# Attention and two MLP layers on one core: another order of reads, loads and first products, and the second product six tiles behind

## The chip, the cores and the metric

The kernel runs on one core of a Trainium2 chip. The metric is the device time of one execution in microseconds: 915.09 before the change, the median of three runs (912.17 to 916.41).

## The reference

Three parts, one after the other. Attention with 2 batches, 8 heads, 768 positions and head size 64:

```python
scores = scale * np.matmul(q, k.transpose(0, 1, 3, 2))
is_global = pos[None, :] < int(n_global)                  # 8
is_local = (rel >= 0) & (rel < int(n_local))              # 96
dist = np.where(is_global & ~is_local, float(n_local), np.abs(rel))
scores = np.where(is_global | is_local, scores - slopes * dist, -1e9)
a = softmax(scores)                                       # over the keys
x = (a @ v), heads side by side                           # 1536 x 512
```

Then an MLP, `h = x @ w_in` (512 to 2048), `g = h * tanh(softplus(h))`, `x2 = g @ w_out`. Then four experts, each `relu(x2 @ w1[e]) @ w2[e]` (512 to 1024 to 512), weighted by normalized `domain_probs` and added.

## The kernel before

**Precision.** The large products are made of fp16 halves: a matrix is scaled by a power of two and split into a high and a low fp16 part, and a product is three matmuls (high x high, high x low, low x high). The scale needs a bound of the largest absolute value, so v, w_in and w_out are each read once for it before they are split.

**Attention.** There are 8 pairs of heads, 12 units in each (6 query tiles of 128 rows, 2 heads). A unit's keys are only the band: the tile before, its own and 32 global columns, 288 columns from the third query tile on, 128 and 256 in the first two. For a unit TensorE makes scores (L540, for two units at a time, three units ahead of use), VectorE adds the distance table and finds the row's extreme (`biased`, L1074, two units ahead), ScalarE takes the exponential (`expo`, L824, two ahead), TensorE transposes (`turn`, L566), ScalarE copies out a high half (L858), VectorE makes the low half (L1184), and TensorE multiplies with the values (`pv`, L585, two units behind). VectorE's `output` divides by the row sums in three small steps per half pair. `fill` (L497) transposes q and k of the next pair, ScalarE copies them out. Every engine's order is written out by hand in `pair`; engines meet at semaphores alone.

Beside this, at steps counted as `at` = 12 x pair + unit: VectorE reads |v| of one pair per unit of pair 0 (`value_step`, L1155). ScalarE reads |w_in| in eight pieces of 1024 columns at steps 21 to 28 and |w_out| at 33 to 40 (`weights_sum`, L841), as a sum of absolute values, which bounds the maximum. GpSimd then splits both matrices (`split_all`, from L745). x of the first 512 tokens is transposed during pairs 4 to 7 (`turn_x`, L505; ScalarE L893 and VectorE L1169 make the halves).

**Head.** SyncE loads the bounds, q and k of pair 0, v of pair 0, q and k of pair 1, then the other v. VectorE writes the identity, tests the bounds, and builds the distance table of 672 columns in eight steps (`distances` and two more, L1040 to L1052). The scores wait for all four copies of q and k of pair 0.

**First MLP.** 1536 tokens in 3 groups of 512, 16 tiles of 128 hidden columns: 48 steps T. In step T TensorE makes the first product of tile T (12 matmuls, `first_product`, L635) into one of four PSUM banks and, LAG = 4 tiles behind, the second product of tile T - 4 (12 matmuls, L658) into the other four. Between them stands the activation: ScalarE's exponential of T (L939), VectorE L1297, L1299, L1303, ScalarE's logarithm and exponential of T - 1 (L953, L955), VectorE L1315, L1317 for T - 1, GpSimd's product (L790), ScalarE's high half and VectorE's low half (L947, L1309) of T - 2. The hidden halves live in a ring of 8 tiles. The groups 1 and 2 of x are transposed in steps 0 and 2, before the first second product, through the banks that the second products use. When a group is done, ScalarE copies x2 out of PSUM (`take_x2`, L911); TensorE's next group waits for it. In ScalarE's order this copy stands at the start of step T = LAG + 16 x group:

```python
for T in range(STEPS + LAG):
    taken = x2_due(T, 0)
    if taken and taken[1] == 0:
        take_x2(taken[0])
```

After step 47 the loop's first products are those of expert 0.

Of the kernel before, what the change touches and what calls it, by code (L numbers as in the profile page):

```python
# [13 lines left out]
P = 128  # L14
# [22 lines left out]
def program(nc, q, k, v, n_global, n_local, w_in, w_out, probs, w1, w2, out):  # L37
# [35 lines left out]
    with ExitStack() as ctx:  # L73
# [103 lines left out]
        dist_b, key_b, loc_b = (scratch(BAND_COLS) for _ in range(3))  # L177
# [5 lines left out]
        rel_b, glo_b = dist_b, tmp[:, 3 * BAND_COLS:4 * BAND_COLS]  # L183
# [56 lines left out]
        w_piece = sem("w_piece")  # L240
# [53 lines left out]
        LAG = 4  # L294


        TURN_AT = {0: 1, 2: 2}
# [21 lines left out]

        W_LOAD_AT = UNITS + 6  # L320
# [16 lines left out]
        FILL = [(j, t) for j in range(2) for t in (range(HEAD), range(HEAD, QT))]  # L337
# [38 lines left out]
        def run_attention(eng, first, pair, rest):  # L376
# [18 lines left out]
            with eng.If(banded == 1):  # L395
                run(True)
                rest()
            with eng.Else():
                run(False)
                rest()  # L400
# [79 lines left out]
        def _(pe):  # L480
            def fill(i, slot, k, banded):
# [14 lines left out]
                for n, t in enumerate(tiles):  # L496
                    last = pe.transpose(psum(k if m_0 else 3, P, n * P), nat[slot][j][:, t * P:(t + 1) * P], ident[:])  # L497
# [10 lines left out]
            def score_parts(i, slot, u, banded):  # L508
# [3 lines left out]
                if u == 0:  # L512

                    pe.wait_ge(tr_out, FILLS * (2 * i + slot + 1))
# [73 lines left out]

            def pair(i, slot, banded):
                for u in range(UNITS):  # L590
# [34 lines left out]
            def rest():  # L625

                pe.wait_ge(o_ready, 2 * PAIRS + 2)

                def split_product(dst, lhs, rhs, chunks, fresh=None):

                    for c in range(chunks):
                        if fresh is not None:
                            fresh(c)
                        for n, (a, b) in enumerate(((0, 0), (0, 1), (1, 0))):
                            last = pe.matmul(dst, lhs(c, a), rhs(c, b), start=(c == 0 and n == 0),  # L635
                                             stop=(c == chunks - 1 and n == 2))
                    return last

                def first_product(T):

                    g, f = divmod(T, FT)
                    if T >= 4:
                        pe.wait_ge(b_ready, T - 3)
                    split_product(psum(T % 4), lambda c, s: w_in_s[:, s, c, f * P:(f + 1) * P],
                                  lambda c, s: xs(g, c, s), DC).then_inc(h_psum, 1)
# [51 lines left out]
                pe.wait_ge(x_ready, DC)  # L697
                pe.wait_ge(w_split, 1)
                for T in range(STEPS + LAG):
                    if T < STEPS:  # L700
# [3 lines left out]
                    if T in TURN_AT:  # L704
                        pe.wait_ge(x_ready, DC * TURN_AT[T])
# [13 lines left out]
            pe.wait_ge(ident_ready, 1)  # L719
            for k in range(FILLS):  # L720
# [85 lines left out]
        def _(act):  # L806
# [27 lines left out]
            def weights_sum(n, c):  # L834
# [6 lines left out]
                act.activation(scaled[:], src[:, c * PIECE:(c + 1) * PIECE], ACT.Abs,  # L841
                               accum_out=wpieces[:, c:c + 1]).then_inc(w_piece, 1)
# [7 lines left out]
            def pair(i, slot, banded):  # L850
                for u in range(UNITS):
# [28 lines left out]
                if not banded and not after(i, slot):  # L880
# [3 lines left out]
                    for c in range(PIECES):  # L884
# [11 lines left out]
            def rest():  # L896
# [79 lines left out]
            for k in range(FILLS):  # L976
                copy_out(0, 0, k, k)
# [4 lines left out]
        def _(dve):  # L982
# [23 lines left out]

            dve.wait_ge(bounds_in, 32)
# [15 lines left out]
            def weights_part(n, c):  # L1023

                if c in (0, PIECES // 2):
# [394 lines left out]
```

## Time and profile before

| | us |
|---|---|
| median of three runs | 915.09 |
| the profiled execution, time | 915.88 |
| its span, first to last instruction | 913.8 |
| TensorE busy in it | 873.1 |
| VectorE busy | 506.8 |
| ScalarE busy | 315.7 |
| GpSimd busy | 266.0 |

PE is TensorE's matmuls, PEld its weight loads, DVE VectorE, ACT ScalarE, POOL GpSimd, SP SyncE. A line number is that of the code above. Busy time is the time in which an engine works on an instruction; where an engine idles the trace tells how long and which instruction ended it. The attention takes the first 154 us, the first MLP to 423 us, the experts the rest.

### The profile page before, as it was taken

The page shows a single profiled execution, that of the slowest core. Times are in us where ns is not written, and L with a number is a line of the kernel's source. Part 1 is how long each engine was busy: PE and PEld are TensorE (multiplying, and loading weights), DVE is VectorE, ACT ScalarE, POOL GpSimd, SP SyncE. Part 2 cuts the span into 40 slices and gives each one's busy share as a digit, 9 for nine tenths or more (in the row PEclk, how much of TensorE's full clock was granted, in tenths as well). Part 3 has the DMA queues.
Part 4 walks back from the last instruction along what each step waited for, and adds up shares of the span by engine and source line. Part 5 has one row for each costly group of instructions (what it writes and reads, how often), then busy time and mean ns, then how long its engine had stood idle before and what let it go on. Part 6 is the DMA issues. An engine that isn't in the chain of part 4 may idle for free.

```text
span 913.8 us, 12568 instructions
## 1 busy us (share of the span) xinstructions
PE 873.1 (96%) x4884; PEld 441.3 (48%) x4884; DVE 506.8 (55%) x1016; ACT 315.7 (35%) x591; POOL 266.0 (29%) x218
## 2 busy tenths in 40 slices
PE   3878998999999999999999999999999999999998
PEld 3766786444444444444444444444444444444443
DVE  7855876999999999996642225322134322212121
ACT  3699885545454555454030111101020101101020
POOL 1266994122222232320009500059000193000000
PEclk8798999999999999999999999999999999999999
DMA  9762340000000000202000400000400000000001
GB/s 220 242 220 55 82 156 1 1 1 1 0 1 10 1 0 1 78 18 93 4 6 0 151 34 0 7 1 2 182 1 0 6 0 0 1 24 23 34 12 49
DMA packets 52005, 39.20 MB, mean 43 GB/s; under 512 B 40816, under 2 KB 41712, under 8 KB 51440
## 3 DMA queue, kind: packets, MB, share of 16 engines
q1 hardware_dynamic: 49888, 34.31, 12.5%
q10 hardware_dynamic: 2064, 4.19, 1.3%
q8 instruction: 31, 0.51, 0.3%
q14 instruction: 22, 0.18, 0.1%
HBM read 35.35 MB, written 3.15 MB: 42 GB/s over the span
## 4 chain that ended last, share of the span: by engine, by line
PE 69%; DVE 21%; ACT 7%; issue 2%; DMA 0%; POOL 0%; DVEq 0%; SPq 0%; ACTq 0%
PE bank L635 58%; PE bank L658 5%; DVE tmp L1299 4%; DVE tmp L1317 3%; PE bank L540 2%; DVE xT L1315 2%; DVE tmp L1297 2%; PE bank L566 2%; DVE tmp L1303 2%; ACT scaled L841 2%; PE bank L585 1%; DVE hid L1309 1%; ACT tmp L824 1%; ACT tmp L858 1%; ACT tmp L953 1%
## 5 line engine op out<-in xcount | busy, mean ns | idle before, releaser
L927 ACT ACTIVATE hid<-bank 128x512 f16<-128x512 f32 x96 | 57.3, 596 | 410.6 <-PE bank L635 410.6
L635 PE MATMUL bank<-xT,wA 128*128 128x512 f16 (+1 forms) x864 | 196.2, 381 | 1.1 <-DVE acc L1114 1.1
L1290 DVE SCALAR_TENSOR_TENSOR hid<-bank,hid 128x512 f16<-128x512 f32 x96 | 66.4, 692 | 172.3 <-ACT hid L927 172.3
L658 PE MATMUL bank<-hid,wB 128*128 128x512 f16 x576 | 132.2, 379 | 4.4 <-ACT acc L911 2.6
L635 PEld LDWEIGHTS bank<-xT,wA 128*128 128x128 f16 x864 | 84.8, 98 | 103.7 <-issue 2.2
L790 POOL TENSOR_TENSOR tmp<-tmp 128x512 f32<-128x512 f32 x48 | 70.1, 1460 | 198.2 <-DVE tmp L1317 198.2
L635 PE MATMUL bank<-wA,hid 128*128 128x512 f16 x576 | 125.3, 379 | 0.0
L635 PE MATMUL bank<-xT,wB 128*128 x576 | 125.3, 379 | 0.0
L635 PE MATMUL bank<-wB,hid 128*128 128x512 f16 x576 | 125.3, 379 | 0.0
L745 POOL TENSOR_SCALAR stage<-stage,sc 128x1024 f32<-128x1024 f32 x32 | 35.9, 1120 | 252.8 <-DVEq L1283 240.8
L1366 DVE SCALAR_TENSOR_TENSOR acc<-bank,pg,acc 128x512 f32<-128x512 f32 x36 | 27.0, 751 | 131.7 <-PE bank L635 131.7
L658 PEld LDWEIGHTS bank<-hid,wB 128*128 128x128 f16 x576 | 56.1, 98 | 73.0 <-DVE hid L1309 3.6
L635 PEld LDWEIGHTS bank<-wA,hid 128*128 128x128 f16 x576 | 56.4, 98 | 67.9
L635 PEld LDWEIGHTS bank<-xT,wB 128*128 128x128 f16 x576 | 56.4, 98 | 68.0
L635 PEld LDWEIGHTS bank<-wB,hid 128*128 128x128 f16 x576 | 56.4, 98 | 68.0
L947 ACT ACTIVATE hid<-tmp 128x512 f16<-128x512 f32 x48 | 30.2, 630 | 107.8 <-POOL tmp L790 106.0
L1184 DVE SCALAR_TENSOR_TENSOR tmp<-bank,tmp 128x384 f16<-128x384 f32 (+2 forms) x96 | 47.0, 490 | 30.5 <-ACT tmp L858 29.4
L635 PE MATMUL bank<-xT,hid 128*128 (+1 forms) x288 | 63.3, 379 | 0.0
L824 ACT ACTIVATE tmp<-tmp 128x288 f32<-128x288 f32 (+2 forms) x96 | 48.7, 507 | 20.3 <-DVE tmp L1074 18.8
L566 PE MATMUL bank<-ident,tmp 128*128 128x128 f32 x240 | 47.4, 299 | 6.0 <-DVE tmp L1184 3.3
L1299 DVE SCALAR_TENSOR_TENSOR tmp<-tmp 128x512 f32<-128x512 f32 x48 | 48.4, 1007 | 1.6
L540 PE MATMUL bank<-hid 64*128 64x256 f32 (+2 forms) x320 | 39.7, 360 | 9.1 <-DVE tmp L1074 8.2
(110 smaller groups left out, 930.6 us busy)
## 6 DMA issues: line engine op xcount, KB each, us to landing
stage<-in_moe_w SPq DMA_DIRECT2D x8, 2048.0 KB, 9.1
stage<-in_moe_w_in SPq DMA_DIRECT2D x1, 4096.0 KB, 14.2
wB<-in_moe_w_out ACTq DMA_DIRECT2D x1, 4096.0 KB, 15.9
hid<-in_q SPq DMA_DIRECT2D x16, 192.0 KB, 3.2
hid<-in_k SPq DMA_DIRECT2D x16, 192.0 KB, 3.4
xT<-in_v SPq DMA_DIRECT2D x8, 384.0 KB, 5.1
out_y<-acc SPq DMA_DIRECT2D x12, 256.0 KB, 2.0
rows<-max SPq DMA_DIRECT2D x4, 128.0 KB, 4.2
```

What stands on the lines that cost most here:

```text
L540: last = pe.matmul(*parts[a][n], start=True, stop=True)
L566: last = pe.transpose(dst[:, b * P:(b + 1) * P], src[:, b * P:(b + 1) * P], ident[:])
L635: last = pe.matmul(dst, lhs(c, a), rhs(c, b), start=(c == 0 and n == 0), stop=(c == chunks - 1 and n == 2))
L658: last = pe.matmul(psum(4 + d), w_out_s[:, a, f // 2, f % 2, d * P:(d + 1) * P], hv[:, T % RING, b, :], start=(f == 0 and n == 0), stop=(f ...
L745: pool.tensor_scalar(tmp, src, scale, 1.0, ALU.mult, ALU.mult).then_inc(w_part, 1)
L790: pool.tensor_tensor(g_t[T % 4], g_t[T % 4], r_t[T % 2], ALU.mult).then_inc(g_ready, 1)
L824: act.activation(t, t, ACT.Exp, bias=nmax[:, u:u + 1], scale=-1.0).then_inc(p_ready, 1)
L927: act.activation(hv[:, f, 0, :], psum(f % 4), ACT.Relu).then_inc(f_hi, 1)
L947: act.activation(hv[:, m % RING, 0, :], g_t[m % 4], ACT.Copy).then_inc(h_hi, 1)
L1184: dve.scalar_tensor_tensor(pt[:, 1], src, P_SCALE, pt[:, 0], ALU.mult, ALU.subtract).then_inc(pT_dve, 1)
L1290: dve.scalar_tensor_tensor(hv[:, f, 1, :], psum(f % 4), 0.0, hv[:, f, 0, :], ALU.max, ALU.subtract).then_inc(f_ready, 1)
L1299: dve.scalar_tensor_tensor(n, u, 2.0, u, ALU.add, ALU.mult).then_inc(n_ready, 1)
```

## The change

The distance table takes four instructions instead of eight, with one further instruction on the relative distances and the three memsets moved ahead of the wait for the bounds. The transposes of pair 0 come as q and k of the first four tiles, then of the last two, in other banks, and the first scores wait for the first two copies alone. TensorE gets 13 products of the identity before the first transposes and 3 after the first scores, whose output nobody reads. VectorE makes the biased scores of unit 2 and reads |v| of pair 1 before v0's low half. |v| of pairs 3, 5 and 7 is read by ScalarE, that of 2, 4 and 6 by VectorE. Of the eight pieces of |w_in| and |w_out| ScalarE reads the first, third, ..., VectorE the others, at the same steps. In the last pair, behind the turns of units 9, 10 and 11, TensorE makes the first product of tile 0 and half of that of tile 1. LAG becomes 6, and the groups 1 and 2 of x are transposed in steps 1 and 3. In this shortened diff a comment names the function.

```diff
-        dist_b, key_b, loc_b = (scratch(BAND_COLS) for _ in range(3))
+        dist_b, key_b = (scratch(BAND_COLS) for _ in range(2))
...
-        LAG = 4
-        TURN_AT = {0: 1, 2: 2}
+        LAG = 6
+        TURN_AT = {1: 1, 3: 2}
+        EARLY = [(0, (0, 1)), (0, (2, 3)), (1, (0, 1))]
...
+        V_SUMS = list(range(3, PAIRS, 2))
...
-        FILL = [(j, t) for j in range(2) for t in (range(HEAD), range(HEAD, QT))]
+        FILL = [(j, t) for t in (range(HEAD), range(HEAD, QT)) for j in range(2)]
...
# fill
-                    last = pe.transpose(psum(k if m_0 else 3, P, n * P), ...
+                    last = pe.transpose(psum(4 + k if m_0 else 3, P, n * P), ...
# score_parts
-                if u == 0:
-
+                if banded and before(i, slot) is None:
+                    if u in (0, 2 * HEAD):
+                        pe.wait_ge(tr_out, 2 if u == 0 else FILLS)
+                elif u == 0:
                     pe.wait_ge(tr_out, FILLS * (2 * i + slot + 1))
...
+            def keep_busy(times):
+
+                for _ in range(times):
+                    pe.matmul(psum(3, P), ident[:], ident[:], start=True, stop=True)
+
             def first(banded):
                 if banded:
                     scores_of_two(0, 0, 0)
                     scores_of_two(0, 0, 2)
+                    keep_busy(3)
...
+            def first_product(T, only=None):
+
+                g, f = divmod(T, FT)
+                if T >= 4:
+                    pe.wait_ge(b_ready, T - 3)
+                last = split_product(psum(T % 4), lambda c, s: w_in_s[:, s, c, f * P:(f + 1) * P],
+                                     lambda c, s: xs(g, c, s), DC, only=only)
+                if not only or DC - 1 in only:
+                    last.then_inc(h_psum, 1)
# pair, TensorE
                         if ahead and u % 2:
                             scores_of_two(*ahead)
+                        if not after(i, slot) and u >= UNITS - len(EARLY):
+                            n = u - (UNITS - len(EARLY))
+                            if n == 0:
+                                pe.wait_ge(x_ready, DC)
+                                pe.wait_ge(w_split, 1)
+                            first_product(*EARLY[n])
                         if behind:
                             pv(*behind, banded)
# rest, TensorE
-                pe.wait_ge(o_ready, 2 * PAIRS + 2)
...
                 for T in range(STEPS + LAG):
-                    if T < STEPS:
+                    if banded and T < 2:
+                        if T:
+                            first_product(1, (2, 3))
+                    elif T < STEPS:
                         first_product(T)
                     else:
                         expert_first(0, 0, T - STEPS)
                     if T in TURN_AT:
+                        pe.wait_ge(o_ready, 2 * PAIRS + 2)
                         pe.wait_ge(x_ready, DC * TURN_AT[T])
...
             pe.wait_ge(ident_ready, 1)
+            keep_busy(13)
...
# weights_sum, ScalarE
-                if n + c:
-                    act.wait_ge(w_piece, PIECES * n + c)
+                act.wait_ge(w_sum, PIECES // 2 * n + c // 2 + len(V_SUMS))
...
+            def values_sum(n):
+
+                act.wait_ge(v_loaded[n], 16)
+                if V_SUMS.index(n):
+                    act.wait_ge(w_sum, V_SUMS.index(n))
+                act.activation(scaled[:, 0:PV], v_all[:, n * PV:(n + 1) * PV], ACT.Abs,
+                               accum_out=vpart[:, n:n + 1]).then_inc(w_sum, 1)
# pair, ScalarE
-                        if start <= at < start + PIECES:
+                        if at - start in range(0, PIECES, 2):
...
+                    if at + 1 in V_SUMS:
+                        values_sum(at + 1)
# VectorE, before the wait for the bounds
+            dve.wait_ge(iotas, 3)
+            dve.scalar_tensor_tensor(rel_b, rel_b, -1.0e9, rel_b, ALU.mult, ALU.max)
+            for s in s_b:
+                last = dve.memset(s[:, 2 * P + GLOBAL_COLS:3 * P], 0.0)
+            link(last)
...
# band_tables
-                distances(link, rel_b, key_b, loc_b, glo_b)
-                link(dve.tensor_scalar(loc_b, loc_b, -1.0, 1.0e9 * 2 ** H / SCALE, ALU.add, ALU.mult))
-                dve.scalar_tensor_tensor(dist_b, rel_b, -1.0 / SCALE, loc_b, ALU.mult, ALU.add).then_inc(band_ready, 1)
+                link(dve.tensor_scalar(key_b, key_b, bf[:, 0:1], -1.0e9 * 2 ** H / SCALE, ALU.is_ge, ALU.mult))
+                link(dve.scalar_tensor_tensor(key_b, rel_b, bf[:, 1:2], key_b, ALU.is_ge, ALU.mult))
+                link(dve.tensor_scalar(rel_b, rel_b, bf[:, 1:2], -1.0 / SCALE, ALU.min, ALU.mult))
+                dve.tensor_tensor(dist_b, rel_b, key_b, ALU.add).then_inc(band_ready, 1)
# matrix_step
+                    first = W_SUMS[case].get(n)
+                    if first is not None and at - first in range(1, PIECES, 2):
+                        weights_part(n, at - first)
# pair, VectorE
-                    elif ahead:
+                    elif ahead and ahead != (0, 0, 2):
                         biased(*ahead, banded)
# attention, VectorE
+                if is_banded:
+                    biased(0, 0, 2, is_banded)
                 dve.wait_ge(v_amax, 1)
                 make_scale(chain(scale_step), scale_cols(SC_V0))
                 dve.sem_inc(v_scale, 1)
+                value_step(0)
                 values_low(0)
-                pair(0, 0, is_banded, value_step)
+                pair(0, 0, is_banded, lambda u: u and value_step(u))
...
# expert_group, VectorE
-                            x2_max(NG - 1, f - begun)
+                            for c in range(DC):
+                                if f == min(begun + c, ET - 1):
+                                    x2_max(NG - 1, c)
```

## Rows read from the trace of the kernel before

**Rows 1.** The page: busy tenths in 40 slices of 22.85 us.

```profile
PE   3878998999999999999999999999999999999998
DVE  7855876999999999996642225322134322212121
POOL 1266994122222232320009500059000193000000
```

**Rows 2.** Stretches: length, busy us of PE, PEld, DVE, ACT, POOL, clock, DMA.

```profile
60.00:80.00 20.00, 13.85 (x173) 11.16 (x171) 11.96 (x48) 18.79 (x45) 7.62 (x9) 0.97 0.39 103
...
300.00:400.00 100.00, 97.84 (x455) 44.17 (x453) 95.73 (x137) 55.27 (x88) 30.62 (x19) 1.00 0.06 22
```

**Rows 3.** Timeline of the head: start us, us, engine, line, instruction.

```profile
6.61 0.51 DVE L1040 TENSOR_SCALAR tmp<-tmp 128x672 f32<-128x672 f32 x1 [1.04 <-issue]
7.63 2.79 PE L497 MATMUL bank<-ident,hid 128*128 128x128 f32 x12 [7.63 <-DMA hid<-in_k]
...
12.34 0.86 DVE L1052 SCALAR_TENSOR_TENSOR tmp<-tmp 128x672 f32<-128x672 f32 x1
13.87 0.29 DVE L1074 CUSTOM_DVE_ANT_0 tmp<-bank,tmp 128x128 f32<-128x128 f32 x1 [0.23 <-DVE tmp L1384]
```

**Rows 4.** SyncE's issue of v, and v's time to landing.

```profile
9.09 9.72 SPq L420 DMA_DIRECT2D xT<-in_v  x7
...
DMA to landing us min/median/max: 3.9/5.1/5.4
```

**Rows 5.** Timeline, VectorE in pair 0.

```profile
17.98 1.02 DVE L1144 SCALAR_TENSOR_TENSOR xT<-xT,sc 128x768 f16<-128x768 f32 x1 [1.06 <-ACT xT L832]
...
22.01 0.45 DVE L1074 CUSTOM_DVE_ANT_0 tmp<-bank,tmp 128x288 f32<-128x288 f32 x1
```

**Rows 6.** A stretch, and TensorE's timeline before it.

```profile
14.00:16.00 2.00, 1.78 (x7) 1.14 (x8) 1.41 (x5) 0.80 (x2) 0.25 (x1) 0.53 1.14 260
...
14.22 1.22 PE L540 MATMUL bank<-hid 64*128 64x256 f32 x4 [2.78 <-DVE tmp L1074]
```

**Rows 7.** Timeline, ScalarE and VectorE while |w_in| is read.

```profile
64.17 0.50 ACT L858 ACTIVATE tmp<-bank 128x384 f16<-128x384 f32 x1
64.54 0.55 ACT L824 ACTIVATE tmp<-tmp 128x288 f32<-128x288 f32 x1
64.70 0.56 DVE L1184 SCALAR_TENSOR_TENSOR tmp<-bank,tmp 128x384 f16<-128x384 f32 x1 [0.94 <-ACT tmp L858]
65.18 0.45 DVE L1074 CUSTOM_DVE_ANT_0 tmp<-bank,tmp 128x288 f32<-128x288 f32 x1
...
66.01 0.50 ACT L858 ACTIVATE tmp<-bank 128x384 f16<-128x384 f32 x1
```

**Rows 8.** Line 1028 alone: count, ns min/median/max, first and last start.

```profile
L1028 DVE TENSOR_REDUCE wpieces<-stage x32: 1208/1210/1220, 194.2 to 699.6; 128x1 f32<-128x1024 f32 x32
```

**Rows 9.** Timeline, TensorE and VectorE at the end of attention.

```profile
148.47 0.52 PE L566 MATMUL bank<-ident,tmp 128*128 128x128 f32 x3
...
152.53 0.43 PE L585 MATMUL bank<-xT,tmp 128*128 128x65 f16 x9 [0.49 <-DVE tmp L1184]
154.04 4.43 PE L635 MATMUL bank<-xT,wA 128*128 128x512 f16 x12 [1.08 <-DVE acc L1114]
154.08 0.16 DVE L1266 TENSOR_TENSOR sc<-sc 128x1 f32<-128x1 f32 x1
```

**Rows 10.** Timeline, VectorE and TensorE in the first MLP.

```profile
159.29 0.43 DVE L1297 TENSOR_SCALAR tmp<-tmp 128x512 f32<-128x512 f32 x1 [5.05 <-ACT tmp L939]
...
257.60 2.75 PE L658 MATMUL bank<-hid,wB 128*128 128x512 f16 x12 [0.47 <-ACT acc L911]
...
338.09 0.69 DVE L1317 SCALAR_TENSOR_TENSOR tmp<-xT,tmp 128x512 f32<-128x512 f32 x1
342.79 2.75 PE L658 MATMUL bank<-hid,wB 128*128 128x512 f16 x12 [2.15 <-ACT acc L911]
...
349.24 0.69 DVE L1317 SCALAR_TENSOR_TENSOR tmp<-xT,tmp 128x512 f32<-128x512 f32 x1
```

More of the change, by code:

```diff
@@ L396, in run_attention @@
                 run(True)
-                rest()
+                rest(True)
             with eng.Else():
                 run(False)
-                rest()
+                rest(False)
         block = ctx.enter_context(nc.Block())
@@ L587, in pv, with split_product @@
                 last.then_inc(pv_done, 1)
+            def split_product(dst, lhs, rhs, chunks, fresh=None, only=None):
+                for c in only or range(chunks):
+                    if fresh is not None:
+                        fresh(c)
+                    for n, (a, b) in enumerate(((0, 0), (0, 1), (1, 0))):
+                        last = pe.matmul(dst, lhs(c, a), rhs(c, b), start=(c == 0 and n == 0),
+                                         stop=(c == chunks - 1 and n == 2))
+                return last
+            def first_product(T, only=None):
[6 more added lines that the diff above has]
+                    last.then_inc(h_psum, 1)
             def pair(i, slot, banded):
@@ L623, in pair, with rest @@
                     share_max(1)
-            def rest():
-                pe.wait_ge(o_ready, 2 * PAIRS + 2)
[L629 to L645, printed above, removed]
+            def rest(banded):
                 def second_product(T):
@@ L883, in pair @@
                     act.wait_ge(w_max, 1)
-                    for c in range(PIECES):
+                    for c in range(0, PIECES, 2):
                         weights_sum(1, c)
@@ L893, in x_high, with rest @@
                 act.activation(xs(g, c, 0), psum(x_bank(g, c)), ACT.Copy).then_inc(x_hi, 1)
-            def rest():
+            def rest(banded):
                 def x2_high(g, c):
@@ L1023, in weights_part @@
             def weights_part(n, c):
[L1025 removed]
+                if n < 2 and c == 1:
+                    dve.wait_ge(w_out_loaded if n else w_loaded, 16)
+                if n >= 2 and c in (0, PIECES // 2):
                     dve.wait_ge(w2_loaded if c else w1_loaded, 16 * (n - 1))
                 at = c * PIECE
[L1028 removed]
+                src = w_out_raw if n == 1 else stage
+                dve.tensor_reduce(wpieces[:, c:c + 1], src[:, at:at + PIECE], AX_X, ALU.max,
                                   apply_absolute_value=True).then_inc(w_piece, 1)
@@ L1150, in value_step @@
             def value_step(u):
-                if u + 1 < PAIRS:
-                    n = u + 1
+                n = u + 1
+                if n < PAIRS and n not in V_SUMS:
                     dve.wait_ge(v_loaded[n], 16)
@@ L1378, in _ @@
             with dve.If(banded == 1):
-                link = chain(table_step)
-                dve.wait_ge(iotas, 3)
-                band_tables(link)
+                band_tables(chain(table_step))
                 dve.wait_ge(band_ready, 1)
-                for s in s_b:
-                    last = dve.memset(s[:, 2 * P + GLOBAL_COLS:3 * P], 0.0)
-                link(last)
                 attention(True)
@@ L1392, in _ @@
                 dve.sem_inc(tables_free, 1)
+                for c in range(1, PIECES, 2):
+                    weights_part(1, c)
                 weights_max(1)
```

27 lines of the change are left out of this document (15 added, 12 removed).

## The prediction

> **What bounds the kernel now.** I read the page's slices first [rows 1]: TensorE is at nine tenths or more in nearly every slice after the seventh (from about 160 us), so most of the span can't shrink. Only the first sixth, the attention, has room on TensorE, and VectorE is at nine tenths from 160 to 410 us as well. The stretches [rows 2] say who bounds each stage. From 60 to 80 us ScalarE is busy 18.79 of 20 us and TensorE 13.85: this is where |w_in| and |w_out| are read.  From 300 to 400 us, inside the first MLP, VectorE has 95.73 and TensorE 97.84 of 100: two engines at their limit, and a change that lets one run ahead waits for the other soon. From 420 us on (experts) TensorE's slices are full but for the last. So the change is worth what it does to the head (0 to 20 us), the two weight readings, the passage from attention to MLP at 150 to 160 us, and the MLP's pace.
>
> **Head: short table, loads in another order.** Before, eight table instructions of 672 columns fill VectorE from 6.61 to 13.20 us, and the first biased scores start at 13.87 [rows 3]. After, one of them (and three memsets) stands before the wait for the bounds; it ends 0.3 us after the bounds are there, so the rest starts near 6.9. Four are left: two like L1040 (0.54 with its gap) and two like L1052 (0.9), 2.9 us: done at 9.8. Then the scores bind: the twelve transposes run 7.63 to 10.42 [rows 3], the scores need the first eight and two copies, and come at about 11.2. Gain 2.6 at the first biased scores. The value path follows: reduce of |v0|, all-reduce, scale. The next bound is a transfer. VectorE now reads |v1| before it writes v0's low parts; v1 is issued at 9.09 us (seven issues in 9.72 us, 1.39 each) and a v lands 5.1 us after its issue [rows 4]: 14.2. Then 0.9 for the read (three quarters of the 1.21 of a 1024-column one [rows 8]), 1.15 for the low parts (1.02 at 17.98 [rows 5]) and their ones, 0.25 and 0.45 for the unit's low half and the biased scores of unit 3, 0.2 for unit 1's, 0.85 for |v2|: the biased scores of unit 4 start at 18.0 where they start at 22.01 now [rows 5]. Head: **-4.0**. Bounds: -2.6 (only what the first scores gain) and -6.0 (if TensorE also keeps its full clock to unit 8, next paragraph).
>
> The thirteen dummy products take 13 x 0.23 us (twelve transposes in 2.79 [rows 3]), 3.3 to 6.3 us, while TensorE waits for q and k: they delay nothing. Three more after the first scores cost at most 0.7 us, in a wait for VectorE. Whether they help is the clock: it is full at first and falls to 0.53 in 14 to 16 us [rows 6], after TensorE had nothing to do for the 2.78 us before 14.22 [rows 6]. After the change TensorE still waits for the values from about 12.5 to 16.5, so I expect the fall again, and cost it at nothing. The Trainium skill (TensorE: Matmul & The Clock Gate, "What's actually happening") says that the default state is throttled and activity releases it; by that rule dummies that fill the wait would hold 2.4 GHz. The trace agrees that a fall follows a pause; these dummies end before the pause that matters, and by the rule too nothing would change, unless that pause has become short enough, which is the -6.0 end.
>
> **|v| in turn.** VectorE drops three reads of 0.85 us, ScalarE gets three of about 0.83 (0.75 of the 1.04 of a weight piece, and its accumulator). What counts is how they chain, and the next part shows that two engines in turn take as long as one. Pair 0: **0**, between -1.5 and +1.
>
> **|w_in| and |w_out| in turn.** A piece now sits on ScalarE at odd-numbered steps and on VectorE at even ones, eight steps per matrix. Before, ScalarE alone sets a step: from the copy at 64.17 to the one at 66.01, 1.84 us, two steps 3.68 [rows 7]; VectorE waits 0.94 in each. After, within two steps: copy of unit u to its VectorE half 0.53 (64.17 to 64.70), that half 0.48 (64.70 to 65.18), VectorE's piece 1.13 (1.21 of L1028 [rows 8] less the 0.08 that the next instruction overlaps, as 0.56 of L1184 takes 0.48), the biased scores of u+3, which stand behind it in VectorE's order, 0.45 and 0.04 to ScalarE; then ScalarE's exponential of u+3 and, behind it, its own piece, 1.47 (64.54 to 66.01), and only then the copy of u+2. Sum 4.10 against 3.68: +0.42, because the queues of both engines are in order, each blocks the other in turn and nothing runs side by side. Four such rounds, and in the first an output step of about 0.48 stands between piece and biased scores: 4 x 0.42 + 0.48 = 2.16 per matrix, two matrices: **+4.3**. The bounds: if the halves did overlap, VectorE's load decides: 2 x (0.48 + 0.49) + 1.13 = 3.07, 0.6 less than 3.68 per round, -4.9 for eight rounds, but TensorE's and the fills' work bring that to some -3; the upper end is +5. POOL's splits follow the scales and end in the slice of 137 to 160 us [rows 1], and the second is wanted only with the second products, some 20 us later: a shift of 4 us is hidden.
>
> **First MLP products in the last pair.** 18 products (1.5 tiles) at 0.215 us (455 in 97.84 us [rows 2]), 3.87 us, go behind the last three turns. A turn adds 0.36 and a value product 0.27 (0.52 and 0.43 listed [rows 9], less the 0.16 that the next overlaps). In order from 148.47: three turns 1.08, products 3.87, four value products 1.1, so unit 11's value product starts at 154.6, not 152.53: **+2.1** for VectorE's outputs. TensorE's pause before the products goes, and with it the slow first tile: twelve products in 4.43 us at 154.04 [rows 9] instead of 2.6. Who profits is VectorE: its first MLP instruction waited for that tile until 159.29 [rows 10]. Now only the scales of the rest (154.08 + 0.16 [rows 9]) and 0.82 us of exponential (158.47 to 159.29) stand before it: 155.06. **-4.2**. Together VectorE starts the MLP 2.1 us earlier.
>
> **Six tiles behind.** Before, VectorE has full slices from 159.29 to past the first hand-over [rows 1], and TensorE is held twice by ScalarE's copy of a finished x2 group out of PSUM: 0.47 us at 257.60 and 2.15 at 342.79 [rows 10]. That copy stands in ScalarE's order at step T = LAG + 16 (and + 32), behind the hidden tile T - 3, which needs VectorE's last instruction on it (L1317). At the second hand-over this is 338.09, and TensorE goes on at 342.79, 4.70 later. With LAG 6 the copy stands two steps later, behind VectorE's L1317 of 349.24: 11.15 us more of VectorE's work (two steps, one with an expert piece). TensorE in turn has done two more first products by then, 24 x 0.215 = 5.2 us. What is late next is VectorE: 11.15 - 5.2 = **+6.0**. Nothing after it takes this back, since TensorE has no pause after 342.79. Bounds: 0 and below (-2.6, both stalls gone) if VectorE weren't the bound; above, 8, if the long stall at the first hand-over (some 6 us, which the second hand-over's slack absorbs) lowers the clock.
>
> **Sum** against the profiled execution's 915.88 (its span 913.80 and 2.08 around it): -4.0 + 0 + 4.3 + 2.1 - 4.2 + 6.0 = +4.2, so 920.1. The median is 0.8 below that execution: 919.3.
>
> **Rivals.**
> Side by side (faster): the readings overlap, -3 for +4.3, and the head keeps its clock, -5 for -4: 919.3 - 7.3 - 1 = 911, or lower with one more gain. For it: VectorE waits 0.94 in each step of the readings. Against: the order of both queues.
> TensorE sets the MLP (faster): what the longer distance is for. Both stalls go, -2.6 for +6.0: 919.3 - 8.6 = 910.7. It decides once VectorE reaches the second hand-over 6 us sooner than I have it; against it is that VectorE's slices are full up to there. With the rival above too: 903.
> Clock and cover lost (slower): the stall at the first hand-over drops TensorE to 1.2 GHz and the second leaves less slack than I think, 4.43 - 2.6 = 1.8 us once (the price at 154.04), and the head gains 2.6 only, 1.4: 919.3 + 3.2 = 922.5. It decides when TensorE rests longer than the second stall is.
> The change does nothing: gains and losses cancel: 915.
>
> **Numbers.** The forecast's own mechanisms 0.42, side by side 0.16, TensorE sets the MLP 0.12, slower clock 0.18, cancelling 0.12. Within 0.5% (4.6 us, about what a measurement of this kernel can tell from no change) is 910.5 to 919.7, and the forecast lies near its upper edge: half of its chance is beyond it. Faster 0.19, same 0.41, slower 0.40. Range: from the faster rivals' 909 to 925 (slower rival and +2).
>
> **What would show it.** Right: biased scores of unit 4 near 18 us; two steps of a weight reading about 4.1 us apart, VectorE and ScalarE both idle in turn; VectorE's L1297 counterpart first at 2 us earlier against the end of attention plus the shift of its start; no pause of VectorE from there to the first hand-over; TensorE idle about 6 us at the first copy of x2 and 3 us at the second, waiting for ScalarE. Wrong: TensorE without those two idles, or weight readings of under 3.5 us per two steps.

## The result: 920.4 us, half a percent slower, and the profile after

After the change the kernel takes 920.44 us (median of 9 runs, 918.70 to 921.23) against 915.11 (9 runs, 912.17 to 916.58). The ratio is 1.0055 with a 95% interval of 1.0042 to 1.0068. The forecast was 919.3, in a range of 909 to 925.

The page after the change, in the order of [rows 1], with the clock beside them: busy tenths in 40 slices, here of 22.98 us.

```profile
PE   6878999899979998999999999999999999999998
DVE  6766887999988999984642214322135322212121
POOL 1357992222222222230008600059000194000000
PEclk8887999999989999999999999999999999999999
```

TensorE's eighth slice (161 to 184 us) has lost a tenth, its twelfth (253 to 276 us) has lost two tenths and a tenth of clock, its sixteenth (345 to 368) one; before they stood at nine. All three lie inside the first MLP: the eighth where TensorE waits for the halves of x ahead of the first second product, the other two at the two hand-overs of x2 (the places where ScalarE copies a finished group out of PSUM and TensorE's next group waits for it). TensorE's slices of the experts are unchanged.

**Head.** The timeline after (start us, us, engine, line, instruction; lines have moved: L1119 is the old L1074, L500 the old L497). These answer to [rows 3] to [rows 5].

```profile
3.37 4.89 PE L558 MATMUL bank<-ident 128*128 128x128 f32 x26 [3.37 <-DVE ident L1038]
3.70 0.86 DVE L1041 SCALAR_TENSOR_TENSOR tmp<-tmp 128x672 f32<-128x672 f32 x1 [0.39 <-POOL tmp L761]
8.10 1.47 PE L500 MATMUL bank<-ident,hid 128*128 128x128 f32 x12
8.93 0.86 DVE L1097 TENSOR_TENSOR tmp<-tmp 128x672 f32<-128x672 f32 x1
10.63 0.29 DVE L1119 CUSTOM_DVE_ANT_0 tmp<-bank,tmp 128x128 f32<-128x128 f32 x1 [0.84 <-PE bank L545]
13.97 0.95 DVE L1203 TENSOR_REDUCE vpart<-xT 128x1 f32<-128x768 f32 x1 [0.62 <-DMA xT<-in_v]
14.85 1.01 DVE L1192 SCALAR_TENSOR_TENSOR xT<-xT,sc 128x768 f16<-128x768 f32 x1
17.52 0.45 DVE L1119 CUSTOM_DVE_ANT_0 tmp<-bank,tmp 128x288 f32<-128x288 f32 x1
```

The table is done at 9.8, the first biased scores start at 10.63 instead of 13.87, VectorE waits for |v1|'s transfer until 13.97 (`DMA xT<-in_v`), and the biased scores of unit 4, the first with 288 columns, start at 17.52, 4.5 us sooner. The all-reduce of |v| starts at 28.15 against 32.28, and at the end of pair 0 ScalarE's copies come 4.1 us sooner.

**Reading |w_in|.** ScalarE (L889 copies, L848 exponentials, L864 pieces) and VectorE (L1233 halves, L1070 pieces, L1119 biased scores) in one round of two steps, against [rows 7]:

```profile
57.48 0.37 ACT L889 ACTIVATE tmp<-bank 128x256 f16<-128x256 f32 x1
58.17 0.38 ACT L889 ACTIVATE tmp<-bank 128x256 f16<-128x256 f32 x1
58.22 1.21 DVE L1070 TENSOR_REDUCE wpieces<-stage 128x1 f32<-128x1024 f32 x1
59.45 0.42 DVE L1119 CUSTOM_DVE_ANT_0 tmp<-bank,tmp 128x288 f32<-128x288 f32 x1
59.91 0.53 ACT L848 ACTIVATE tmp<-tmp 128x288 f32<-128x288 f32 x1 [1.36 <-DVE tmp L1119]
60.81 1.06 ACT L864 ACTIVATE scaled<-stage 128x1024 f32<-128x1024 f32 x1
61.86 0.48 ACT L889 ACTIVATE tmp<-bank 128x384 f16<-128x384 f32 x1
```

VectorE's piece starts at 58.22, beside ScalarE's copy, so far as hoped. But the biased scores of the next unit stand behind it (59.45), ScalarE waits 1.36 us for them (59.91), and only then comes ScalarE's own piece (60.81), for which VectorE waits in turn. From copy to copy over two steps it is 4.38 us here (57.48 to 61.86, with one copy-out of a fill); run 6 below has the same two steps with ScalarE alone. The shift of ScalarE's copies, unit by unit, is -4.05 us up to step 21, -2.04 at steps 31 to 34, +0.58 at steps 43 to 45, and +0.9 in the pairs 4 to 7 (a minus is sooner than before the change): the two readings and their scales cost 5.0 us.

**End of attention and first MLP**, against [rows 9] and [rows 10]; L606 is the old L635 and L675 the old L658, L1349 and L1369 the old L1297 and L1317, L944 the old L911:

```profile
149.36 0.53 PE L577 MATMUL bank<-ident,tmp 128*128 128x128 f32 x3
149.72 1.46 PE L606 MATMUL bank<-xT,wA 128*128 128x512 f16 x6
154.88 0.99 PE L596 MATMUL bank<-xT,tmp 128*128 128x65 f16 x27
156.98 0.16 DVE L1318 TENSOR_TENSOR sc<-sc 128x1 f32<-128x1 f32 x1
157.96 0.43 DVE L1349 TENSOR_SCALAR tmp<-tmp 128x512 f32<-128x512 f32 x1 [0.81 <-ACT tmp L972]
...
176.36 2.76 PE L675 MATMUL bank<-hid,wB 128*128 128x512 f16 x12 [1.17 <-DVE xT L1218]
...
260.80 0.69 DVE L1369 SCALAR_TENSOR_TENSOR tmp<-xT,tmp 128x512 f32<-128x512 f32 x1
264.68 2.03 ACT L944 COPY acc<-bank 128x512 f32<-128x512 f32 x4
265.40 4.93 PE L675 MATMUL bank<-hid,wB 128*128 128x512 f16 x12 [5.98 <-ACT acc L944]
...
348.63 0.69 DVE L1369 SCALAR_TENSOR_TENSOR tmp<-xT,tmp 128x512 f32<-128x512 f32 x1
353.34 2.75 PE L675 MATMUL bank<-hid,wB 128*128 128x512 f16 x12 [2.72 <-ACT acc L944]
```

The products stand behind the turns (149.72), VectorE's last scale comes at 156.98 instead of 154.08, its first MLP instruction at 157.96 instead of 159.29. TensorE waits for ScalarE's copy 5.98 us at the first hand-over and 2.72 at the second, where it waited 0.47 and 2.15.

Stretches around the first hand-over (length, busy us of PE, PEld, DVE, ACT, POOL, clock, DMA share, GB/s):

```profile
259.00:266.00 7.00, 1.02 (x4) 0.29 (x3) 6.76 (x11) 4.68 (x9) 1.27 (x1) 0.79 0.00 1
266.00:268.00 2.00, 2.00 (x6) 0.68 (x5) 1.30 (x3) 1.36 (x4) 1.27 (x1) 0.50 0.04 1
268.00:270.00 2.00, 2.00 (x7) 0.70 (x6) 1.86 (x4) 1.82 (x3) 0.00 (x0) 0.54 0.00 0
270.00:300.00 30.00, 30.00 (x141) 13.58 (x140) 25.70 (x50) 13.37 (x21) 6.62 (x6) 1.00 0.07 7
```

And from the timeline, VectorE's instruction behind it:

```profile
273.67 0.43 DVE L1349 TENSOR_SCALAR tmp<-tmp 128x512 f32<-128x512 f32 x1 [1.43 <-ACT tmp L972]
```

The granted clock is 0.50 and 0.54 in the two stretches behind the pause, that is 1.2 GHz for some 4 us, and twelve matmuls take 4.93 us where they otherwise take 2.75. VectorE, which was the late one, now waits 1.43 us: for ScalarE's exponential, which itself waits for TensorE's first product.

### The profile page after: what moved, and what is told of

The parts are those of the page before. It is cut to its first block, busy times and chain, and to the rows that moved or that the text cites. A ratio compares the mean times of both kernels' runs of the same rounds, so it can differ in the third digit from the quotient of the medians.

```text
span 919.3 us, 12631 instructions
## 1 busy us (share of the span) xinstructions
PE 879.8 (96%) x4916; PEld 447.5 (49%) x4916; DVE 506.8 (55%) x1018; ACT 310.9 (34%) x581; POOL 263.5 (29%) x218
## 4 chain that ended last, share of the span: by engine, by line
PE 74%; DVE 16%; ACT 5%; issue 3%; SPq 1%; DMA 0%; POOL 0%; DVEq 0%; ACTq 0%
PE bank L606 60%; PE bank L675 7%; DVE tmp L1351 3%; PE bank L545 3%; PE bank L577 2%; DVE tmp L1369 2%; DVE xT L1367 2%; DVE tmp L1349 2%; PE bank L596 2%; DVE wpieces L1070 1%; DVE tmp L1355 1%; DVE hid L1361 1%; PE bank L500 1%; ACT tmp L986 1%; ACT tmp L848 1%
## 5 line engine op out<-in xcount | busy, mean ns | idle before, releaser
L606 PE MATMUL bank<-xT,wA 128*128 128x512 f16 (+1 forms) x864 | 194.6, 379 | 0.0
L675 PE MATMUL bank<-hid,wB 128*128 128x512 f16 x576 | 134.3, 383 | 9.9 <-ACT acc L944 8.7
L606 PEld LDWEIGHTS bank<-xT,wA 128*128 128x128 f16 x864 | 84.5, 98 | 100.6 <-DVE tmp L1355 0.2
L606 PE MATMUL bank<-wA,hid 128*128 128x512 f16 x576 | 125.3, 379 | 0.0
L606 PE MATMUL bank<-xT,wB 128*128 x576 | 125.3, 379 | 0.0
L606 PE MATMUL bank<-wB,hid 128*128 128x512 f16 x576 | 125.3, 379 | 0.0
L814 POOL TENSOR_TENSOR tmp<-tmp 128x512 f32<-128x512 f32 x48 | 67.3, 1403 | 201.2 <-DVE tmp L1369 201.2
L675 PEld LDWEIGHTS bank<-hid,wB 128*128 128x128 f16 x576 | 56.6, 99 | 80.2 <-DVE hid L1361 9.6
L606 PEld LDWEIGHTS bank<-xT,wB 128*128 128x128 f16 x576 | 56.4, 98 | 68.0
L606 PEld LDWEIGHTS bank<-wB,hid 128*128 128x128 f16 x576 | 56.3, 98 | 68.0
L606 PEld LDWEIGHTS bank<-wA,hid 128*128 128x128 f16 x576 | 56.3, 98 | 68.0
L1233 DVE SCALAR_TENSOR_TENSOR tmp<-bank,tmp 128x384 f16<-128x384 f32 (+2 forms) x96 | 47.0, 490 | 30.9 <-ACT tmp L889 29.8
L606 PE MATMUL bank<-xT,hid 128*128 (+1 forms) x288 | 63.6, 379 | 0.0
L848 ACT ACTIVATE tmp<-tmp 128x288 f32<-128x288 f32 (+2 forms) x96 | 48.3, 505 | 27.3 <-DVE tmp L1119 26.0
L606 PEld LDWEIGHTS bank<-xT,hid 128*128 128x128 f16 x288 | 28.2, 98 | 34.0
```

The source lines that it names most:

```text
L675: last = pe.matmul(psum(4 + d), w_out_s[:, a, f // 2, f % 2, d * P:(d + 1) * P], hv[:, T % RING, b, :], start=(f == 0 and n == 0), stop=(f ...
L814: pool.tensor_tensor(g_t[T % 4], g_t[T % 4], r_t[T % 2], ALU.mult).then_inc(g_ready, 1)
L848: act.activation(t, t, ACT.Exp, bias=nmax[:, u:u + 1], scale=-1.0).then_inc(p_ready, 1)
L1233: dve.scalar_tensor_tensor(pt[:, 1], src, P_SCALE, pt[:, 0], ALU.mult, ALU.subtract).then_inc(pT_dve, 1)
```

## Experiments

Each ran five rounds against the kernel before, on the same chip. The chip was another for each group of runs (1, 4, 6 and 7; 2, 3, 5 and 8; 9, 10 and 11; 12), and the kernel before had medians of 914.6 to 916.2 in them, so a microsecond or so between runs of two groups means nothing; each ratio is against the kernel before of its own group.

**1. LAG 4 alone.**

```diff
-        LAG = 6
+        LAG = 4
```

> The changed kernel with LAG 4 again, all else as changed. Theory (the hand-over of x2 makes six tiles cost 6): TensorE starts the second products at 176.4 as after the change, reaches the first hand-over about 259.3 and the copy is there already (VectorE's L1369 of tile 17 near 251, 3.3 us for the rest), the second hand-over comes at 342.4 against 347.9 for the same work before and 353.3 after; no idle over 1 us at either. Time 920.4 - 5.8 = 914.6. Rival (TensorE sets the MLP and the distance of six pays): 920.4 or more, up to 923, with TensorE waiting for hidden tiles instead.

Measured: 918.84 us (918.54 to 919.55), ratio 1.0039 (1.0024 to 1.0053). Slower than the expected 914.6 by 4 us. TensorE:

```profile
176.53 5.30 PE L675 MATMUL bank<-hid,wB 128*128 128x512 f16 x12 [6.33 <-DVE xT L1218]
346.70 2.75 PE L675 MATMUL bank<-hid,wB 128*128 128x512 f16 x12 [1.45 <-ACT acc L944]
```

It has two first products fewer to do before the halves of group 2 are there, and stands 6.33 us for them, and the twelve matmuls after take 5.30. I had taken the time of the first second product from the run with six tiles, where seven first products lie ahead of it, and compared it with the wrong amount of work. At the first hand-over there is no pause, as expected; at the second, which I had at 342.4 with under 1 us of waiting, there is one of 1.45 and TensorE goes on at 346.70. So the run as a whole missed, and it doesn't settle what the distance costs. LAG and the place of the transposes belong together, so this undid half of one edit.

**2. LAG 4 and the transposes in steps 0 and 2.**

```diff
-        LAG = 6
-        TURN_AT = {1: 1, 3: 2}
+        LAG = 4
+        TURN_AT = {0: 1, 2: 2}
```

> LAG 4 with the transposes of groups 1 and 2 in steps 0 and 2, as before the change; all else as changed. In the run with LAG 4 alone TensorE stood 6.33 us before the first second product and then ran at the lower clock, since the halves of group 2 came one VectorE step later (step 3) than with LAG 4 before. Theory: with both undone the first second product starts near 172.8, the second hand-over near 341.5, against 342.8 before and 353.3 after: 920.4 - 5.2 - 1.3 = 913.9. Rival (six tiles cost nothing by themselves, which the 918.8 of LAG 4 alone speaks for): 918 to 920.

Measured: 915.17 us (913.59 to 917.64), ratio 1.0009 (0.9995 to 1.0023). The first second product starts at 172.12, the hand-overs are at 255.88 and 341.05, 12.3 us before the one of the changed kernel, of which 5.2 is work not yet done. The two constants undone give back 5.3 us by the medians (4.8 if each is taken against its own kernel before), and the kernel is level with the one before. The time is 1.3 us above the forecast although the second hand-over is no later than forecast (341.5); the twelve matmuls at 341.05 take 4.44 us, 1.7 more than the usual 2.75, which is enough for it.

**3. Six tiles in the kernel before.**

```diff
-        LAG = 4
+        LAG = 6
```

(and the last group's maxima at `min(begun + c, ET - 1)`, as in the change.)

> The kernel before with LAG 6 alone. Theory: the start of the second products is no longer held (177.4 us, seven first products done), but TensorE stands some 6.7 us at the first hand-over and 2.5 to 4 at the second, which comes near 353.5 instead of the 347.9 for the same work: 915.7 + 5.5 = 921.2. Rival (a longer distance alone pays or is neutral; the early products of the change brought the loss): 913 to 916.

Measured: 923.48 us (920.73 to 924.23), ratio 1.0093 (1.0071 to 1.0115). TensorE and VectorE:

```profile
267.55 5.28 PE L658 MATMUL bank<-hid,wB 128*128 128x512 f16 x12 [7.11 <-ACT acc L911]
276.59 0.43 DVE L1297 TENSOR_SCALAR tmp<-tmp 128x512 f32<-128x512 f32 x1 [2.20 <-ACT tmp L939]
356.26 2.75 PE L658 MATMUL bank<-hid,wB 128*128 128x512 f16 x12 [2.72 <-ACT acc L911]
```

The longer distance alone makes the kernel before slower by 8.9 us, where I had 5.5 (the time is 2.3 above the expected 921.2; the kernel before was 1.1 faster in this group than the 915.7 I had started from). The stalls are 7.11 and 2.72 us, and the second hand-over is at 356.26, 2.8 later than forecast. What the trace has in between is behind the first stall: twelve matmuls take 5.28 us, and VectorE waits 2.20 us, again for an exponential. That this is the whole excess was not tested.

**4. The copies of x2 two steps earlier in ScalarE's order, LAG still 6.**

```diff
-                    taken = x2_due(T, 0)
-                    if taken and taken[1] == 0:
+                    taken = x2_due(T, -2)
+                    if taken and taken[0] < NG - 1 and taken[1] == 0:
```

> LAG stays 6, but ScalarE's copies of x2 (first two groups) stand two steps earlier in its order, at steps 20 and 36. Theory: what costs is not the distance but the place of the copy. The copy then hangs on VectorE's L1369 of tile 17 and 33 again; but ScalarE waits there for TensorE, which ends the group near 256.7, some 2.4 us, and that delays VectorE once. First hand-over near 259.5, second near 344.6 instead of 353.3: 920.4 - 8.7 = 911.7, TensorE idle together under 3 us instead of 8.7. Rival (VectorE's total work bounds the MLP, wherever the copy stands): within 1 us of 920.4. Rival (ScalarE's wait costs VectorE as much as is won): 916 to 918.

Measured: 909.55 us (907.73 to 911.75), ratio 0.9938 (0.9921 to 0.9956). ScalarE's copy and TensorE at the first hand-over, from the timeline:

```profile
253.06 2.53 ACT L944 COPY acc<-bank 128x512 f32<-128x512 f32 x4
257.39 2.75 PE L675 MATMUL bank<-hid,wB 128*128 128x512 f16 x12
```

And the stretches of the MLP, with the columns as above:

```profile
180.00:260.00 80.00, 80.00 (x373) 36.24 (x372) 75.47 (x106) 41.52 (x68) 19.86 (x16) 1.00 0.00 1
260.00:270.00 10.00, 10.00 (x48) 4.56 (x47) 9.63 (x16) 4.90 (x8) 2.72 (x2) 1.00 0.01 0
```

The four copies start at 253.06 and take 2.53 us together, since they wait for the last banks of the group one by one; TensorE's next group follows at 257.39 without a pause. TensorE is busy in every microsecond of these stretches, and of those to 360 us. ScalarE's wait, which I had priced at 2.4 us, is some 0.5 (2.53 against the 2.03 of the copies at 264.68), and the time is 2.2 us below the expected 911.7. This is the experiment that names the cause: the distance of six is worth having, the copy's place was not moved along with it.

**5. The same in the kernel before** (LAG 6 and the copies two steps earlier, nothing else of the change but the last group's maxima).

```diff
-        LAG = 4
+        LAG = 6
...
-                    taken = x2_due(T, 0)
-                    if taken and taken[1] == 0:
+                    taken = x2_due(T, -2)
+                    if taken and taken[0] < NG - 1 and taken[1] == 0:
```

> The kernel before with LAG 6 and ScalarE's copies of x2 two steps earlier in its order. Theory: no hand-over stall; TensorE starts its second products at 177.4 with seven first products done, and from there is never idle: for the same work it is 342.8 + 5.2 - (177.4 + 32 x 5.18) = 4.8 us earlier: 915.7 - 4.8 = 910.9. Rival (ScalarE waits at the copy and VectorE falls behind): 914 to 917.

Measured: 910.99 us (907.57 to 911.92), ratio 0.9955 (0.9941 to 0.9968). The time is the expected 910.9 to 0.1 us, but that is partly luck: the gain over the kernel before is 3.6 us in this group, and I had 4.8, from a higher start. From 152.3 us to 400 TensorE has no pause.

**6. All pieces on ScalarE.**

```diff
-                        if at - start in range(0, PIECES, 2):
+                        if start <= at < start + PIECES:
                             weights_sum(n, at - start)
```

(VectorE's pieces at these steps go, and the semaphore counts follow.)

> All eight pieces of |w_in| and |w_out| are read by ScalarE again, at the same steps; all else as changed. Theory (two in-order queues block each other in turn): two steps of a reading fall from 4.1 to 3.7 us, attention ends 5.0 us sooner (4.3 from my sum, 5.0 from the copies' shifts in the trace), and all that follows shifts: 920.4 - 5.0 = 915.4. Rival (the readings cost nothing, the loss is elsewhere, as in TensorE's half clock around 80 us): within 1.5 us of 920.4. Rival (turns do help): above 921.

Measured: 915.56 us (913.52 to 917.12), ratio 0.9999 (0.9989 to 1.0009): 4.9 us less than the changed kernel, where the copies' shifts said 5.0 and my sum 4.3. In its trace the two steps shown above run from the copy at 56.48 to the one at 60.42:

```profile
56.48 0.38 ACT L889 ACTIVATE tmp<-bank 128x256 f16<-128x256 f32 x1
60.42 0.50 ACT L889 ACTIVATE tmp<-bank 128x384 f16<-128x384 f32 x1
...
153.39 0.43 DVE L1350 TENSOR_SCALAR tmp<-tmp 128x512 f32<-128x512 f32 x1 [0.81 <-ACT tmp L972]
```

3.94 us, with the fill's copy, against 4.38: 0.44 less, where the forecast for one round was 0.42. VectorE starts the MLP at 153.39, 4.57 us sooner.

**7. Both** (4 and 6 together).

> take2early and act_pieces together, LAG 6, the rest as changed. Theory: the two costs are of different stages and add: 920.4 - 8.7 - 5.0 = 906.7, faster than the kernel before by 8.4 us (0.9%). Rival: the second covers part of the first (the MLP absorbs an earlier start, because w_out's split or the copies come late): 910 to 912.

Measured: 905.12 us (903.42 to 905.24), ratio 0.9884 (0.9867 to 0.9900). Less than the changed kernel by 15.3 us, where runs 4 and 6 give back 10.9 and 4.9: the two add, as costs of two stages do.

**8. No first products in the last pair.**

```diff
-        EARLY = [(0, (0, 1)), (0, (2, 3)), (1, (0, 1))]
+        EARLY = []
...
-                    if banded and T < 2:
+                    if banded and T < 0:
```

(and the waits for x and for the split weights, which stood ahead of the early products, stand ahead of the MLP.)

> The changed kernel without first products in the last pair (all of them behind it, not waiting for the last output); all else as changed. Theory: what the last pair loses, 2.0 us, VectorE gains by not waiting for the first tile; without them VectorE's first MLP instruction is at 157.3 if tile 0 runs at 2.4 GHz and 159.1 if at 1.2, against 157.96: time 919.8 to 921.6. Rival (the early products only lengthen the attention): 918.4.

Measured: 920.64 us (920.05 to 921.83), ratio 1.0070 (1.0050 to 1.0090), no different from the changed kernel. The timeline of TensorE and VectorE at the start of the MLP:

```profile
153.07 5.34 PE L606 MATMUL bank<-xT,wA 128*128 128x512 f16 x24
156.65 0.43 DVE L1349 TENSOR_SCALAR tmp<-tmp 128x512 f32<-128x512 f32 x1 [2.13 <-ACT tmp L972]
```

TensorE begins the MLP at 153.07, right behind the last value product, because the wait for the last output has moved to the first transposes; it keeps 2.4 GHz (24 matmuls in 5.34 us), and VectorE starts at 156.65. So the moved wait alone brings what I had credited to the early products. VectorE's start, 1.3 us sooner than in the changed kernel, is not in the time: VectorE waits 0.65 us for the second tile at 159.17, the two hand-overs come 0.6 us sooner (264.81 and 352.69), and the medians show nothing of that.

**9. The version of 7 without first products in the last pair** (the edit of 8 on top of those of 4 and 6).

> The version of 905.1 without first products in the last pair. Theory: as in the changed kernel, nothing or up to 1 us slower: 905.1 to 906. Rival (now that TensorE has no stall later, what it does in the last pair counts in full, 3.9 us of work less the 2 us by which the pair is longer): 907.

Measured: 903.74 us (902.78 to 905.13), ratio 0.9883 (0.9864 to 0.9902). I had expected 905.1 to 906. It can't be told from run 7; slower it is not.

**10. The version of 7 with the transposes in steps 0 and 2.**

```diff
-        TURN_AT = {1: 1, 3: 2}
+        TURN_AT = {0: 1, 2: 2}
```

> The version of 905.1 (LAG 6, copies of x2 two steps earlier, all pieces on ScalarE) with the transposes of groups 1 and 2 in steps 0 and 2. Theory: TensorE's two pauses ahead of the first second product (1.39 and 1.15 us) go, but it waits about 1 us for the last output ahead of step 0's transposes, which the half tile covered: 903.6, between 903 and 905. Rival (VectorE bounds the MLP after all): 905.

Measured: 904.41 us (903.30 to 904.50), ratio 0.9883 (0.9863 to 0.9903). The two pauses ahead of the first second product are gone, one of 1.07 us before step 0's transposes is there, and one of 0.71 at the second hand-over. Not to be told from run 7 either.

**11. No dummy products.**

```diff
-                    keep_busy(3)
...
-            keep_busy(13)
```

> The changed kernel without its 16 dummy products of the identity; all else as changed. The trace after the change has the clock at 1.2 GHz from about 17 to 24 us, before the change from 14 to 27.5. Theory: the early start comes from the short table and the order of VectorE's work; the dummies hold the clock at best until TensorE pauses (13.9 to 16.3 us). Within 1 us of 920.4. Rival (the dummies keep the clock up while the transposes of pair 1 and the first turns run, and the pause then falls shorter): 921.5 to 923.5.

Measured: 919.70 us (918.72 to 921.86), ratio 1.0052 (1.0034 to 1.0071). For the time the 16 products bring nothing. In the head they do something, as TensorE's first transposes without them show:

```profile
7.71 2.79 PE L500 MATMUL bank<-ident,hid 128*128 128x128 f32 x12 [7.71 <-DMA hid<-in_k]
```

In the four traces without dummies (this one, the kernel before, runs 3 and 5) the twelve transposes take 2.79 us; in the ten traces with them they take 1.47 in nine and 1.70 in one. But the 13 dummies take 4.6 to 5.9 us and hold the transposes back to between 7.76 and 9.07, so the first biased scores come at 10.29 to 11.82 with them and at 11.42 without, and behind those the scales and |v1|'s transfer decide: the all-reduce starts at 27.67 to 28.22 with them, and here at 27.94. TensorE's clock in the head of the changed kernel (columns as in the stretches around the first hand-over):

```profile
14.00:16.00 2.00, 0.00 (x0) 0.00 (x0) 1.93 (x4) 1.10 (x4) 0.00 (x0) 1.00 1.21 272
18.00:20.00 2.00, 2.00 (x10) 1.58 (x10) 1.05 (x4) 1.99 (x6) 0.00 (x0) 0.50 1.07 244
22.00:24.00 2.00, 2.00 (x9) 1.54 (x10) 1.10 (x4) 2.00 (x6) 0.00 (x0) 0.50 1.12 256
```

The same columns without the dummy products:

```profile
14.00:16.00 2.00, 1.90 (x11) 1.26 (x9) 1.81 (x4) 1.65 (x4) 0.00 (x0) 1.00 1.26 282
16.00:18.00 2.00, 0.50 (x5) 0.38 (x5) 1.93 (x8) 0.95 (x3) 0.00 (x0) 1.00 1.19 271
20.00:22.00 2.00, 2.00 (x21) 1.87 (x18) 1.80 (x5) 1.67 (x5) 0.00 (x0) 0.50 1.17 266
```

TensorE's pause is at 14 to 16 us with dummies and at 16 to 18 without, and either way the clock is at 1.2 GHz for some microseconds about 20 us. At the very start the clock of these views is no guide: it says 1.00 from 8 to 10 us with and without dummies, where the transposes take 1.47 and 2.79 us, and 1.00 from 14 to 16 without, where eight score matmuls take 1.49 us (14.40), as they do at the granted 0.50 (19.18 after the change).

**12. |v| on VectorE alone.**

```diff
-        V_SUMS = list(range(3, PAIRS, 2))
+        V_SUMS = []
```

(and the scale made without the raised exponent, as before the change.)

> The changed kernel with |v| of pairs 3, 5 and 7 read by VectorE again (seven reads by VectorE, as before the change, and v's scale made as before); all else as changed. Theory (VectorE and ScalarE in turn cost what VectorE alone costs): within 1.5 us of 920.4, and the all-reduce of |v| starts within 1.5 us of the 28.15 us after the change. Rival (as with the pieces of w_in and w_out, turns cost some 0.6 us per round, three rounds): 918.6. Rival (turns help here): 922.

Measured: 920.79 us (918.88 to 921.51), ratio 1.0050 (1.0037 to 1.0064); the all-reduce starts at 27.68 against 28.15, which is within what traces with the same head differ by (27.67 in run 8, 28.22 in run 4). No gain or loss by the turns there can be told.

## Why the prediction was right, point by point

| step | forecast | after, from the two traces | by itself |
|---|---|---|---|
| head | -4.0 | -4.1 at the end of pair 0 (-4.5 at unit 4) | |
| abs(v) in turn | 0 | | run 12: no difference |
| abs(w_in), abs(w_out) in turn | +4.3 | +5.0 | run 6: +4.9 by the medians |
| first products in the last pair | +2.1 | +2.0 | run 8: with the early products and without them the same time |
| VectorE's earlier MLP start | -4.2 | -4.2 (5.21 us from last scale to first instruction, now 0.98) | run 8: the moved wait brings it |
| six tiles behind | +6.0 | +6.7 | run 2: +5.3, with the transposes' place |
| sum | +4.2 | +5.4 (span 913.8 to 919.3: +5.5) | |

The +6.7 is 353.34 against 342.79 + 5.2 for the same work, 5.35, and the 1.33 us by which VectorE started sooner and which are lost by then. The kernel ends later by what the second hand-over was later, as no pause of TensorE's for a copy is added behind it. The interval of the ratio (0.42 to 0.68% slower) reaches down to under half a percent.

**Mis-sized.** The readings in turn cost 5.0 and not 4.3. By the copies' shifts |w_in| cost 2.0, as priced (2.16); |w_out| cost 2.6: between steps 34 and 36, where VectorE makes the scale of w_in ahead of its piece, the copies lost 1.13 where I had 0.90, and behind its last piece 0.59 where I had 0.42. Another 0.35 came at step 48; I did not follow it. The hand-over cost 0.7 more: from VectorE's start in the MLP to the L1369 that the second copy waits for it took 190.67 us (157.96 to 348.63), 0.72 more than the 189.95 to the same tile before (159.29 to 349.24). I had held that the first stall's low clock is covered by slack at the second. VectorE was not slow enough for that; it waited for exponentials 0.70 us at 267.34, 1.43 at 273.67 and twice 0.71 behind that, where before it waited for one once, 0.76 us (259.54). Run 3 shows the same more strongly. That the low clock alone makes the 0.7 is read from the traces, not tested. This was in the rival "clock and cover lost", which was a part of the truth and not the whole.

**Right in size, wrong in reason.** The passage into the MLP gained 2.1 us as forecast, but I wrote that it is the early products which free VectorE. Run 8 has none and VectorE starts 1.3 us sooner still. What frees it is that TensorE no longer waits for the last output before the first tile, which keeps both the time and the clock. That the two lines of the sum came out right is luck to that extent: the early products could have been left out at the same time.

**The head, right in sum, not in parts.** The first biased scores gained 3.2 us and not 2.6. The gap is in the transposes: they took 1.47 us and not 2.79, for I had read the clock as full at first, and the durations say otherwise (run 11). The dummies took 4.89 us and not 13 x 0.23, since each is listed as two instructions (x26), and the transposes started 0.5 us later than before the change (8.10 against 7.63), so "they delay nothing" was wrong too. It did not matter, because VectorE then waits for |v1|'s transfer, which I had at 14.2 and which ended at 13.97. The exponential ahead of VectorE's start in the MLP was at 158.57 before, not 158.47: 0.72 us and not 0.82.

**Rivals.** "Side by side" fell with run 6: the turns cost. "TensorE sets the MLP" fell for this kernel with runs 2 and 3 and came true with run 4, once the copy was moved: I had its worth at 8.6 us against the forecast, and it was 10.9 against the changed kernel. "Cancelling" fell with the interval. The chance for slower by over 0.5% was 0.40, the measured 0.55% is just there.

**The dummies** I had at nothing, since TensorE pauses behind them; for the time run 11 agrees.

**Not settled.** Whether the head's gain is the short table's or the order's was not tried apart. The three versions around 904 us (runs 7, 9 and 10) can't be ranked, nor can their differences among each other be put down to anything.

## What to carry to other kernels

When a software pipeline is made deeper, every step that another engine carries at a fixed distance must be placed anew: here the same deeper pipeline is 8.9 us slower or 3.6 us faster than the shallower one, by one line of ScalarE's order. Work shared between two in-order engines in turn is not shared when each one's next necessary output stands behind its share; add up the loop across both queues first. And when an edit moves a wait and some work at once, test the wait alone.

## What the runs showed of the hardware that I had not expected

The same pause of TensorE need not have the same effect on its clock. After 2.72 us at the second hand-over twelve matmuls took 2.75 us in the changed kernel and 4.01 with all pieces on ScalarE; after 2.74 us they took 4.42 in run 12; after 2.15 us they took 2.75 in the kernel before [rows 10] and after 2.14 us 4.44 in run 2. TensorE's timeline with all pieces on ScalarE:

```profile
347.87 4.01 PE L675 MATMUL bank<-hid,wB 128*128 128x512 f16 x12 [2.72 <-ACT acc L944]
```

And in run 2:

```profile
341.05 4.44 PE L675 MATMUL bank<-hid,wB 128*128 128x512 f16 x12 [2.14 <-ACT acc L944]
```

And in run 12:

```profile
352.04 4.42 PE L675 MATMUL bank<-hid,wB 128*128 128x512 f16 x12 [2.74 <-ACT acc L945]
```

After 5.59 to 7.11 us, seven pauses in as many traces, they took 4.0 to 5.3 us each time. What decides it after the short ones no run here shows. Where the clock fell, the twelve matmuls cost 1.3 to 1.7 us more, and a forecast for this kernel carries that much doubt for each pause of 2 to 3 us.
